# A convolution and expert kernel: the inverse step's imaginary sums, a second V buffer, later routing steps and an earlier gather

## The chip, the core and the metric

The kernel runs on one core of a Trainium2 chip. The metric is the device time of one execution in microseconds (us). Engines are named as in the profile: PE (TensorE, matmuls), DVE (VectorE), ACT (ScalarE), POOL (GpSimd), SP (the engine that issues most of the transfers here).

## What is computed

Eight batches of 3072 rows and 256 columns go through a circular convolution along the rows, done in the frequency domain. All 24576 resulting rows then go through a mixture of eight experts with a capacity each: a row goes to the expert of its largest logit, the first 768 rows of an expert (3072 / 8 * 2) are kept, and every other row of the output is zero.

```python
X = np.fft.rfft(x, axis=1)
Y = X * (filt_r + 1j * filt_i)[None, :, :]
x = np.fft.irfft(Y, n=3072, axis=1).reshape(B * S, D)
logits = x @ w_gate                      # 8 experts
expert_idx = np.argmax(logits, axis=1)
...
for i in range(N):                       # rows in order, capacity 768
    e = expert_idx[i]
    if counts[e] < capacity:
        disp[e, counts[e]] = x[i]
        ...
h = np.maximum(np.einsum('ecd,edf->ecf', disp, w1), 0.0)
y = np.einsum('ecf,efd->ecd', h, w2)
out[i] = gate_w[i] * y[expert_idx[i], pos[i]]      # kept rows only
```

## The kernel before, in words

**Two rounds, of which one counts.** The kernel first treats two and a half batches (t = 0, 1, 2; t = HALF = 2 is half a batch) and then all experts. Only where the experts are not full by then, a second round over the rest follows behind a branch; with this data it does not run.

**A stage** is the work of one t. It has eight steps h = 0 to 7, one for each group of four frequency pairs:

- *forward* (`pe_forward`, L475): 16 small matmuls of `wf` with `z_in` into PSUM banks 4 and 5 (`wide`);
- *multiply* (`dve_multiply`, L791): two DVE products of 128x1024 of `wide` with the filter `fab`, into `prod[:, n % 2, 0]` and `prod[:, n % 2, 1]`. The next forward waits for both (`p_done`), since `wide` is there once;
- *sums* (`dve_sums`, L797 and L799): a subtraction makes the real part in `prod[..., 0, :, 0, :]`, an addition the imaginary part in `prod[..., 0, :, 1, :]`;
- *inverse* (`pe_inverse`, L491) of the step before: 32 matmuls of 64x64 by 64x96 in four quadrants of PE, which accumulate real and imaginary part into PSUM banks 3 and 6 (`back`). It waits for both sums (`m_done`);
- *back* (`act_back`, L698): two ACT copies from `back` into `v_in`.

A matmul of `f32` shows as two records in the trace, so that a forward has 32 and an inverse 64; the transposes show once.

**Between them lies the work on the batch before** (`tok`): *logits* at h = 0 (`pe_logits`, L538), twelve *turns* of V, transposes on PE (`pe_turn_v`, L548) and ACT copies into `x_in` (L713), with *raw* (L558) after the second and *route in* (L569) after the fourth; twelve *products* (`pe_product`, L582) with ACT copies into `y` (L727) and stores of `y` to DRAM (`y_store`); thirty *route steps* on DVE (`dve_route`, steps 0 to 29 along `STEPS_BY`), among them the rank of step 10, which needs two matmuls (`pe_rank`, L593), and the table of step 28, which needs 24 matmuls (`pe_table`, L608) after step 27. The route ends in `dve_tokens` (L954 to L958), the row numbers by which the experts gather.

**Queues.** Every engine runs its instructions in the order of the code. SP issues the stores of `t_out` and `y`, the loads of `z_in` (`z_load`, into one of four buffers), the zeros of the output and the weights (`raw_load`), each behind a wait of its own. `first_raw`, the weights of the first expert, lie over `t_in`, and so does `t_out`.

**After the last stage** (`pe_last`, `act_last`, `dve_last`) the half batch is turned and multiplied. Its six rows of products take PSUM banks 0 to 3 (`place_of_row`); after the fourth comes the turn of the first gathered block (`pe_block_turn`, L646), and after the sixth `free_work` for all banks and then the rank.

**The experts** work through 16 blocks of 384 rows: *up* (L1267, 48 matmuls, into banks 4 to 7), *down* (L1281, 72 matmuls, banks 2 and 3), and before each up the *turn* of its block (L646), whose rows POOL gathers from DRAM (`pool_gather`, L1155). POOL issues in a fixed order: gathers, sends of the output (L1183) and the gates (L1167), with waits between (`pool_after` waits for an up to have come so far).

## Time and profile before

| | us |
|---|---|
| median of three runs | 492.42 |
| lowest and highest | 490.75 and 493.45 |
| the execution that was profiled | 491.62 |
| its span, first to last instruction | 489.8 |
| mean granted clock of TensorE, as a share | 0.989 |

Of the span PE is busy for 455.6 us, DVE for 233.4, ACT for 215.3 and POOL for 186.2. The span falls into a stage 0 (to 73.4 us), stage 1 (to 128), stage 2 (to 174), the last half batch (to 193) and the experts (to 484). A row of the timeline gives start and duration in us, the engine, the line of the code, the tile that is written and the ones that are read, shapes, count, and in brackets how long the engine sat idle before it and for whom.

### The profile page before, as it was taken

What the parts mean: (1) busy time and instruction counts of PE and PEld (TensorE: products, weight loads), DVE (VectorE), ACT (ScalarE), POOL (GpSimd) and SP (SyncE); (2) the same over time, 40 slices, a digit from 0 to 9 for tenths busy, and PEclk for the clock granted to TensorE, in tenths of its full rate; (3) what the DMA queues carried; (4) which work ended last, traced back from release to release, by engine and by line L of the source; (5) the groups of instructions that cost most, each with busy time, mean ns of one, the idle gap of its engine ahead of it and who ended that gap; (6) DMA issues with size and microseconds to landing.
All of it is one profiled execution on the core that took longest, in us unless ns stands there. A gap on an engine that the chain in (4) does not pass through costs nothing.

```text
span 489.8 us, 12096 instructions
## 1 busy us (share of the span) xinstructions
PE 455.6 (93%) x5160; PEld 400.8 (82%) x5160; DVE 233.4 (48%) x382; ACT 215.3 (44%) x402; POOL 186.2 (38%) x159
## 2 busy tenths in 40 slices
PE   5989999997898988999979999999999999999994
PEld 5855557555665574999979999999999999999993
DVE  2085535889399965870652242353134344224300
ACT  2745555452364555622634353455335345423310
POOL 0000000000000060467476787566786457583222
PEclk9999999998999999999989999999999999999998
DMA  8994989759854365733041894411795310970001
GB/s 297 412 403 131 337 257 336 277 206 332 286 166 163 139 225 141 258 98 98 22 141 45 277 387 154 140 44 34 260 399 179 131 43 24 347 276 23 33 34 38
DMA packets 45743, 93.00 MB, mean 190 GB/s; under 512 B 5840, under 2 KB 20848, under 8 KB 45168
## 3 DMA queue, kind: packets, MB, share of 16 engines
q1 hardware_dynamic: 39408, 79.48, 46.3%
q0 software_dynamic: 6272, 12.65, 7.7%
q8 instruction: 43, 0.70, 0.6%
q14 instruction: 20, 0.16, 0.1%
HBM read 46.47 MB, written 45.64 MB: 188 GB/s over the span
## 4 chain that ended last, share of the span: by engine, by line
PE 83%; DVE 10%; issue 3%; DMA 2%; ACT 1%; POOLq 0%; POOL 0%; SPq 0%; DVEq 0%; ACTq 0%
PE psum L1281 29%; PE psum L1267 25%; DVE prod L791 5%; PE psum L491 4%; PE psum L508 4%; PE psum L475 4%; PE psum L548 3%; PE psum L505 3%; PE psum L646 2%; PE psum L582 2%; PE psum L538 2%; PE psum L524 1%; DVE prod L799 1%; PE psum L578 1%; DMA g_in<-y_rows,token 1%
## 5 line engine op out<-in xcount | busy, mean ns | idle before, releaser
L1095 DVE SCALAR_TENSOR_TENSOR hl<-psum,hh 128x384 fp32r<-128x384 f32 x128 | 69.5, 555 | 145.7 <-ACT hh L1046 145.7
L1281 PE MATMUL psum<-w2h,hh 128*128 128x256 f32 x384 | 110.5, 288 | 0.0
L1281 PE MATMUL psum<-w2l,hh 128*128 128x256 f32 x384 | 109.3, 285 | 0.0
L1281 PE MATMUL psum<-w2h,hl 128*128 128x256 f32 x384 | 109.3, 285 | 0.0
L1046 ACT ACTIVATE hh<-psum 128x384 fp32r<-128x384 f32 x128 | 62.1, 492 | 60.8 <-PE psum L1267 60.0
L1267 PE MATMUL psum<-xh,w1h 128*128 128x384 f32 x256 | 86.1, 336 | 1.6 <-DVE hl L1095 1.5
L1267 PE MATMUL psum<-xh,w1l 128*128 128x384 f32 x256 | 85.6, 334 | 0.0
L1267 PE MATMUL psum<-xl,w1h 128*128 128x384 f32 x256 | 85.6, 334 | 0.0
L791 DVE TENSOR_TENSOR prod<-psum,fab 128x1024 f32<-128x1024 f32 x48 | 56.5, 1217 | 49.7 <-PE psum L475 41.9
L1183 POOL DMA_INDIRECT out<-o_out,token x48 | 49.2, 1025 | 74.0 <-ACT o_out L1055 60.1
L1281 PEld LDWEIGHTS psum<-w2l,hh 128*128 128x128 f32 x384 | 74.4, 194 | 0.0
L1281 PEld LDWEIGHTS psum<-w2h,hl 128*128 128x128 f32 x384 | 74.3, 193 | 0.0
L1281 PEld LDWEIGHTS psum<-w2h,hh 128*128 128x128 f32 x384 | 74.3, 193 | 0.0
L1055 ACT ACTIVATE o_out<-psum,o_gate 128x256 f32<-128x256 f32 x48 | 22.8, 476 | 108.3 <-PE psum L1281 108.3
L1155 POOL DMA_INDIRECT g_in<-y_rows,token x48 | 53.5, 1114 | 41.7 <-DVE token L958 26.8
L1167 POOL DMA_INDIRECT o_gate<-gate_rows,token x48 | 48.7, 1014 | 35.1 <-PE psum L1267 21.5
L1146 POOL DMA_DIRECT2D gate_rows<-gate x2 | 1.3, 660 | 145.6 <-DVE carry L893 145.6
L1267 PEld LDWEIGHTS psum<-xh,w1h 128*128 128x128 f32 x256 | 48.1, 188 | 2.5 <-DVE hl L1095 2.1
L1267 PEld LDWEIGHTS psum<-xl,w1h 128*128 128x128 f32 x256 | 48.1, 188 | 0.0
L1267 PEld LDWEIGHTS psum<-xh,w1l 128*128 128x128 f32 x256 | 48.1, 188 | 0.0
L491 PEld LDWEIGHTS psum<-wbi,prod 64*64 64x64 f32 x1536 | 33.9, 135 | 14.6 <-issue 8.8
L491 PE MATMUL psum<-wbi,prod 64*64 64x96 f32 x1536 | 38.9, 249 | 4.8 <-issue 2.3
(111 smaller groups left out, 533.0 us busy)
## 6 DMA issues: line engine op xcount, KB each, us to landing
out<-zero SPq DMA_DIRECT2D x24, 1024.0 KB, 6.2
w_raw<-in_w SPq DMA_DIRECT2D x14, 1024.0 KB, 5.8
x_in<-in_x SPq DMA_DIRECT2D x18, 512.0 KB, 6.7
t_scratch<-t_out SPq DMA_DIRECT2D x24, 256.0 KB, 4.4
z_in<-t_scratch SPq DMA_DIRECT2D x32, 192.0 KB, 3.9
y_rows<-y SPq DMA_DIRECT2D x12, 512.0 KB, 2.8
fab<-in_fab SPq DMA_DIRECT2D x4, 1024.0 KB, 14.4
first_raw<-in_w SPq DMA_DIRECT2D x2, 1024.0 KB, 7.6
```

What stands on the lines that cost most here:

```text
L475: mm = nc.tensor.matmul(wide[q * QR:(q + 1) * QR, a, c, :], wf[part(a), NQ * h + q, c, :], z_in[part(a), n % ZB, q, :], start=True, stop=True)
L491: mm = nc.tensor.matmul(back[q][part(low), at:at + 2 * HR], prod[part(q), n % 2, 0, a, c, d:d + A1], wbi[part(q), j, a, c, :], start=(c == ...
L508: mm = nc.tensor.matmul(work[k][:, :], wa[:, :], x_in[:, c, 2 * h:2 * h + 2, :], start=True, stop=True)
L791: nc.vector.tensor_tensor(prod[:, n % 2, f], wide, fab[:, h, :, f, :].unsqueeze(2).to_broadcast([P, 2, 2, D]), ALU.mult).then_inc(p_done, 1)
L1046: nc.scalar.activation(hh[:, b % 2, f, :], ps[(2, 3, 6, 7)[f % 4]][:, 0:TOK], ACT.Relu).then_inc(hh_done, 1)
L1055: nc.scalar.activation(o_out[:, b % 2, s, :], ps[4 + (b * ST + s) % 2][:, 0:D], ACT.Copy, scale=o_gate[:, b % 4, s:s + 1]).then_inc(o_evac, 1)
L1095: nc.vector.scalar_tensor_tensor(out=hl[:, b % 2, f, :], in0=ps[(2, 3, 6, 7)[f % 4]][:, 0:TOK], scalar=0.0, in1=hh[:, b % 2, f, :].bitcast ...
L1155: nc.gpsimd.indirect_dma_start(out=g_in[:, b % 2, s, :], out_offset=None, in_=yd[0:have], in_offset=bass.IndirectOffsetOnAxis(ap=tokens_of ...
L1167: nc.gpsimd.indirect_dma_start(out=o_gate[:, b % 4, s:s + 1], out_offset=None, in_=gd[0:have], in_offset=bass.IndirectOffsetOnAxis(ap=toke ...
L1183: nc.gpsimd.indirect_dma_start(out=out, out_offset=bass.IndirectOffsetOnAxis(ap=tokens_of(r, b, s), axis=0), in_=o_out[:, b % 2, s, :], in ...
L1267: mm = nc.tensor.matmul(ps[(2, 3, 6, 7)[f % 4]][:, 0:TOK], wt[k][:, h, f * P:(f + 1) * P], xx[:, b % 2, h, :], start=(m == 0), stop=(m == 5))
L1281: mm = nc.tensor.matmul(ps[4 + (b * ST + s) % 2][:, 0:D], hx[:, b % 2, f, s * P:(s + 1) * P], wt[k][:, f, :], start=(f == 0 and m == 0), s ...
```

## The change

Six things are changed at once.

1. *Imaginary sums.* In stages 1 and 2 the groups h = 4, 5 and 6 do not make the imaginary sum on DVE. `prod[..., 0, :, 1, :]` and `prod[..., 1, :, 0, :]` stay apart, and the inverse of these groups has three terms in place of two: 48 matmuls, the third of which adds the second imaginary part with the same `wbi`.
2. *A second V buffer.* Batch t = 1 is written to `v_other`, over `t_in`. Its first copy waits until `t_out` of t = 2 has been stored, and the weights that lie in the same place (`first_raw`, `w1h0`) wait for all turns of that batch.
3. *Turns and products.* The turns move from h = 0 and 1 to h = 1, 2 and 3 (`TURNED`), the products to h = 2 to 6 in both stages (`PRODUCTS`). A product waits for its own turn and no longer for all twelve.
4. *Route steps.* They move later (`STEPS_BY`), the exponential to h = 2, the rank to h = 3 and the table from h = 7 to h = 6. At h = 7 nothing of the route is left.
5. *The last half batch.* Rows 4 and 5 of the products go to banks 4 and 5; the rank goes ahead of them, right behind the first block turn; the wait for the banks is now with the first two parts of the first up, and with the first down.
6. *Queues.* SP loads `z_in` 4 to 6 of the last stage first, then stores two rows of `y`, then loads the first weights, then `z_in` 7; ACT splits the first weights at h = 5 and not at h = 3. POOL gathers block 4 right behind the sends of block 1, ahead of the gates of block 2; before, that gather waited for the second part of the up of block 3.

PE in stage 1, steps 5 to 7, where the chain of waits runs over DVE before the change. L475 is the forward, L491 the inverse, L608 the table, L582 a product. Before:

```order
L475 MATMUL psum<-z_in,wf 32x256 x16
L491 MATMUL psum<-wbi,prod 64x96 x32
L475 MATMUL psum<-z_in,wf 32x256 x16
L491 MATMUL psum<-wbi,prod 64x96 x32
L475 MATMUL psum<-z_in,wf 32x256 x16
L491 MATMUL psum<-wbi,prod 64x96 x32
L608 MATMUL psum<-hot_hi,hot_lo 128x96 x24
L491 MATMUL psum<-wbi,prod 64x96 x32
```

The same steps after (L491, L508, L625 and L599 are forward, inverse, table and product there):

```order
L491 MATMUL psum<-z_in,wf 32x256 x16
L508 MATMUL psum<-wbi,prod 64x96 x48
L599 MATMUL psum<-x_in,wai 128x512 x3
L491 MATMUL psum<-z_in,wf 32x256 x16
L508 MATMUL psum<-wbi,prod 64x96 x48
L625 MATMUL psum<-hot_hi,hot_lo 128x96 x24
L599 MATMUL psum<-x_in,wai 128x512 x3
L491 MATMUL psum<-z_in,wf 32x256 x16
L508 MATMUL psum<-wbi,prod 64x96 x80
```

Six products and the longer inverses stand in these steps now, and the table comes one step earlier; the last row is the inverse of group 6 (48) and that of group 7 (32).

POOL at the start of the experts. L1155 is a gather of three parts, L1183 a send, L1167 the gates. Before:

```order
L1155 DMA g_in<-y_rows,token_79 128x256 x3
L1183 DMA out<-o_out,token_78 24576x256 x3
L1167 DMA o_gate<-gate_rows,token_79 128x1 x3
L1155 DMA g_in<-y_rows,token_79 128x256 x3
L1167 DMA o_gate<-gate_rows,token_79 128x1 x3
```

After (L1179, L1207 and L1191):

```order
L1179 DMA g_in<-y_rows,token_79 128x256 x3
L1207 DMA out<-o_out,token_78 24576x256 x3
L1179 DMA g_in<-y_rows,token_79 128x256 x3
L1191 DMA o_gate<-gate_rows,token_79 128x1 x6
```

The gather of block 4 has moved ahead of the gates of block 2, whose wait stood before it.

PE at the seam from the last half batch to the experts. L578 is a product of the half batch, L646 the turn of the first block, L593 and L594 the rank, L1267 the first up. Before:

```order
L578 MATMUL psum<-x_in,wai 64x512 x8
L646 MATMUL psum<-sq,g_in 128x128 x6
L578 MATMUL psum<-x_in,wai 64x512 x4
L593 MATMUL psum<-lg,tri_half 128x8
L594 MATMUL psum<-lg,sq 128x8
```

After (L595, L663, L610 and L611):

```order
L595 MATMUL psum<-x_in,wai 64x512 x8
L663 MATMUL psum<-sq,g_in 128x128 x6
L610 MATMUL psum<-lg,tri_half 128x8
L611 MATMUL psum<-lg,sq 128x8
L595 MATMUL psum<-x_in,wai 64x512 x4
```

The rank stands ahead of the last two rows of products.


The diff, cut to what changes the order, the work or a wait:

```diff
-EXP_STEP = 1
-RANK_STEP = 2
+EXP_STEP = 2
+RANK_STEP = 3
...
-STEPS_BY = [4, 8, 17, 23, 25, 27, 28, 30]
+STEPS_BY = [0, 5, 10, 22, 25, 28, 30, 30]
...
+TURNED = [0, 0, 4, 8, 12, 12, 12, 12, 12]
+PRODUCTS = [0, 0, 0, 2, 4, 6, 9, 12, 12]
...
+def summed(t, h):
+
+    return t == 0 or h not in (4, 5, 6)
...
+        v_other = sb("v_other", [P, DH, N2, P], over="t_in")
...
         def sp_last_stage(sp, t, r):
-            z_load(sp, t, ZB)
+            for g in range(ZB, NG - 1):
+                z_load(sp, t, g)
+            y_store(sp, t - 1, 0)
+            y_store(sp, t - 1, 1)
             raw_load(sp, r, 0, 0)
             raw_load(sp, r, 0, 1)
-            z_load(sp, t, ZB + 1)
-            z_load(sp, t, ZB + 2)
-            y_store(sp, t - 1, 0)
-            z_load(sp, t, ZB + 3)
-            for c in range(1, products(t - 1) // 2):
+            z_load(sp, t, NG - 1)
+            for c in range(2, products(t - 1) // 2):
                 y_store(sp, t - 1, c)
...
         def pe_inverse(pe, t, j):
...
+            terms = [(0, 0, 0), (0, 1, 1)] if summed(t, j) else [(0, 0, 0), (0, 1, 1), (1, 0, 1)]
             for h in range(DH):
                 for a in range(2):
-                    for c in range(2):
+                    for i, (f, c, to) in enumerate(terms):
...
-                                mm = nc.tensor.matmul(back[q][part(low), at:at + 2 * HR], prod[part(q), n % 2, 0, a, c, d:d + A1],
-                                                      wbi[part(q), j, a, c, :], start=(c == 0), stop=(c == 1))
+                                mm = nc.tensor.matmul(back[q][part(low), at:at + 2 * HR], prod[part(q), n % 2, f, a, c, d:d + A1],
+                                                      wbi[part(q), j, a, to, :], start=(i == 0), stop=(i == len(terms) - 1))
...
         def pe_product(pe, t, i, k):
-            pe.wait_ge(vt_evac, t * 12 + 12 if t != HALF else t * 12 + 2 * i + 2)
+            pe.wait_ge(vt_evac, t * 12 + i + 1 if t != HALF else t * 12 + 2 * i + 2)
...
-                    if h == NG - 1:
+                    if h == NG - 2:
                         pe_table(pe, tok, 7)
-                    for i in products_at(tok, h, t == last - 1):
+                    for i in products_at(r, tok, h, t == last - 1):
                         pe_product(pe, tok, i, next_work("pe"))
...
         def place_of_row(t, i, engine):
-            return 2 + (i - 4) if t == HALF and i >= 4 else next_work(engine)
+            return i if t == HALF and i >= 4 else next_work(engine)
...
                     pe_block_turn(pe, r, 0)
+                    pe_rank(pe, t, 5)
                 pe_product(pe, t, i, place_of_row(t, i, "pe"))
-            for k in range(WORK + 1):
-                free_work(pe, k)
-            if r == 0:
-                pe_rank(pe, t, 5)
+            if r > 0:
+                for k in range(WORK):
+                    free_work(pe, k)
...
         def act_back(act, t, g):
+            if t == 1 and g == 0:
+                for c in range(NCH):
+                    act.wait_ge(t_written[c], 2 * 32)
...
-                nc.scalar.copy(v_in[:, :, :, u:u + 8], back[q].rearrange("p (h x n) -> p h n x", h=DH, n=N2)).then_inc(v_evac, 1)
+                nc.scalar.copy(v_of(t)[:, :, :, u:u + 8], back[q].rearrange("p (h x n) -> p h n x", h=DH, n=N2)).then_inc(v_evac, 1)
...
-                if t == last - 1 and h == 3:
+                if t == last - 1 and h == NG - 3:
                     act_split(act, r, 0, 0)
...
-                                    ALU.subtract).then_inc(m_done, 1)
-            nc.vector.tensor_tensor(prod[:, n % 2, 0, :, 1, :], prod[:, n % 2, 0, :, 1, :], prod[:, n % 2, 1, :, 0, :],
-                                    ALU.add).then_inc(m_done, 1)
+                                    ALU.subtract).then_inc(m_done, 1 if summed(t, h) else 2)
+            if summed(t, h):
+                nc.vector.tensor_tensor(prod[:, n % 2, 0, :, 1, :], prod[:, n % 2, 0, :, 1, :], prod[:, n % 2, 1, :, 0, :],
+                                        ALU.add).then_inc(m_done, 1)
...
                 turned(sp, (FIRST if r == 0 else NB) - 1)
+                if r == 0:
+                    sp.wait_ge(vt_done, 12 * (FIRST - 1))
+                    sp.nop(nofuse=True)
...
             pool_sent(pool, r, 1)
+            pool_gather(pool, r, 4)
             pool_after(pool, r, 2, 6)
             pool_gates(pool, r, 2)
-            pool_after(pool, r, 3, 2)
-            pool_gather(pool, r, 4)
             pool_after(pool, r, 3, 7)
...
                     if n * FT + f >= 4:
                         pe.wait_ge(hl_done, n * FT + f - 3)
+                    elif n == 0 and f < 2:
+                        free_work(pe, 4 + f)
...
             up(1)
+            if r == 0:
+                for k in range(2, 6):
+                    free_work(pe, k)
             down(0, 0)
```

## Rows read from the trace of the kernel before

**Rows 1.** Two stages: PE, PEld, DVE, ACT, POOL busy, granted clock, DMA share, GB/s.

```profile
73.40:128.00 54.60, 46.84 (x1014) 31.91 (x1010) 40.60 (x65) 22.55 (x46) 0.74 (x1) 0.97 0.85 296
128.00:174.00 46.00, 42.64 (x947) 29.62 (x946) 41.69 (x70) 24.61 (x45) 0.57 (x1) 1.00 0.46 157
```

**Rows 2.** The chain that ended last, stage 1: start, duration, what.

```profile
74.49 2.77 PE psum L538 x93
...
77.96 0.41 PE psum L538 x3
...
90.77 1.06 issue
...
117.25 2.03 PE psum L475 x32
...
124.59 1.01 PE psum L475 x29
125.61 1.88 issue
...
128.10 2.76 PE psum L538 x96
```

**Rows 3.** The same chain: what one piece of PE work takes.

```profile
83.79 2.90 PE psum L548 x24
...
97.31 1.48 PE psum L491 x64
98.79 3.63 PE psum L582 x8
...
131.88 1.26 PE psum L558 x12
...
134.05 0.33 PE psum L569 x2
...
217.82 1.07 PE psum L608 x24
```

**Rows 4.** Timeline of DVE, stage 2 and the last half batch.

```profile
146.28 0.17 DVE L891 TENSOR_TENSOR base<-psum,carry 128x8 f32<-128x8 f32 x1
...
148.53 2.35 DVE L791 TENSOR_TENSOR prod<-psum,fab 128x1024 f32<-128x1024 f32 x2
...
151.52 0.69 DVE L799 TENSOR_TENSOR prod<-prod 128x512 f32<-128x512 f32 x1
...
153.63 0.69 DVE L924 TENSOR_TENSOR hot_lo<-digits,pairs 128x1024 bf16<-128x1024 bf16 x1
...
191.47 1.01 DVE L834 TENSOR_TENSOR xl<-psum,xh 128x384 fp32r<-128x384 f32 x2
```

**Rows 5.** The chain at the start of the experts.

```profile
192.03 0.59 ACT y L727
...
192.97 0.36 PE psum L593 x2
193.55 6.35 PE psum L1267 x36
...
247.24 4.93 DMA g_in<-y_rows,token
...
253.09 10.12 PE psum L1281 x72
...
272.18 8.62 PE psum L1281 x72
```

**Rows 6.** Timeline of POOL: the last send of block 1.

```profile
232.78 0.99 POOL L1183 DMA_INDIRECT out<-o_out,token  x1 [0.30 <-issue]
```

**Rows 7.** Timeline of PE: the turn of block 4.

```profile
252.21 0.87 PE L646 MATMUL psum<-sq,g_in 128*128 128x128 f32 x6 [2.50 <-DMA g_in<-y_rows,token]
```

**Rows 8.** Busy time, granted clock (seventh number), DMA share and GB/s behind that turn.

```profile
253.00:256.00 3.00, 3.00 (x19) 3.00 (x19) 1.54 (x3) 2.45 (x3) 2.08 (x4) 0.61 0.16 44
```

**Rows 9.** The page's DMA queues: packets, MB, share of 16 engines.

```profile
q8 instruction: 43, 0.70, 0.6%
```

More of the change, by code:

```diff
@@ L85, in gates_before, with turned_at, products_at @@
     return 16 * sum(2 if k == HALF else 1 for k in range(t))
-def turned_at(h):
+def turned_at(r, h):
+    if r == 0:
+        return range(TURNED[h], TURNED[h + 1])
     return range(6 * h, 6 * h + 6) if h < 2 else range(0)
-def products_at(t, h, last):
+def products_at(r, t, h, last):
+    if r == 0:
+        return range(PRODUCTS[h], PRODUCTS[h + 1])
     if last:
@@ L282, in build @@
         ps = [psum[:, i].rearrange("p k d -> p (k d)") for i in (0, 1, 4, 5, 2, 3, 6, 7)]
-        work = [psum[:, i].rearrange("p k d -> p (k d)") for i in range(WORK + 1)]
+        work = [psum[:, i].rearrange("p k d -> p (k d)") for i in range(6)]
         back = [psum[:, i].rearrange("p k d -> p (k d)")[:, 0:DH * 4 * HR] for i in (3, 6)]
@@ L445, in sp_last @@
                     zeros(sp, n)
-        held = [None] * (WORK + 1)
+        held = [None] * 6
         place_of = {"pe": 0, "act": 0}
@@ L617, in pe_stage @@
                         pe_logits(pe, tok, 1)
-                    for i in turned_at(h):
+                    for i in turned_at(r, h):
                         pe_turn_v(pe, tok, i)
@@ L749, in act_stage @@
                 if tok is not None:
-                    for i in products_at(tok, h, t == last - 1):
+                    for i in products_at(r, tok, h, t == last - 1):
                         act_rows(act, tok, i, next_work("act"))
```

10 lines of the change are left out of this document (7 added, 3 removed).

## The prediction

> **What bounds the kernel now.** I read the stages by their busy time first. In stage 1 PE is busy for 46.8 of 54.6 us and DVE for 40.6, in stage 2 PE for 42.6 and DVE for 41.7 of 46.0 [rows 1]: two engines of nearly equal load that take turns at waiting. The chain of waits says where. Up to about 109 us it runs over PE, then over DVE (multiply, sums, route steps) to the end of stage 1, and over DVE again through nearly all of stage 2. Three more things lie on it. PE pauses three times in stage 1 with "issue" as the reason: 0.70 us ahead of the row at 77.96, 1.06 at 90.77 and 1.88 at 125.61 [rows 2]. One forward at 117.25 takes 2.03 us [rows 2] where 1.0 is usual. Last, at the start of the experts, PE waits 2.50 us for the gather of block 4 [rows 7]. Behind 253 us PE runs without a gap, which leaves up and down alone there; this part of 231 us the change does not touch.
>
> **Prices.** All from one profiled execution of 491.62 us. On PE: a forward about 1.03 (29 of its 32 records in 1.01) [rows 2]; inverse 1.48, four products 3.63 with their start, so 0.86 each, six turns 2.90, so 0.48 each, raw 1.26, route in 0.33, table 1.07 [rows 3]; rank 0.5, from 192.97 to the up at 193.55 [rows 5]; logits 2.76, or 3.88 with the pause in them (2.77 + 0.70 + 0.41) [rows 2]. On DVE: from a multiply to the second sum 3.0 and 0.6 more for that sum (148.53 to 151.52) [rows 4]; route steps 10 to 16 take 2.25 (146.28 to 148.53), steps 17 to 21 1.5 (152.13, where that second sum ends, to 153.63) [rows 4].
>
> **The sums.** A group without the addition saves DVE 0.6 us. Its inverse has 96 records in place of 64: 1.48 x 1.5 = 2.22, so PE pays 0.74. Over six groups that is 3.6 us off DVE and 4.4 us onto PE. It is worth something only where DVE is late. With the new tables six products and the table stand in steps 5 and 6 and make PE the late one there, so I expect no gain from this edit: with plain sums the list below comes out 0.2 us shorter per stage.
>
> **Stage 1, step by step**, from its first forward at 73.47 (74.49 less 1.02). I take for each step the longer of the two engines.
> Step 0: forward and logits with the pause, 4.9. Step 1: forward, four turns, raw, route in, inverse, 1.03 + 1.9 + 1.26 + 0.33 + 1.48 = 6.0. Step 2: forward, four turns, inverse, two products, 6.15. Step 3: the same and the rank, 6.6. Step 4: DVE, which has 3.6 of multiply and sums and 3.75 of route steps behind forward 3, lets forward 5 start 4.6 after forward 4 (PE alone would need 4.25). Step 5: forward, the long inverse 2.22, three products 2.6, 5.85. Step 6: the same and the table, 6.9. Step 7: forward, the multiply 2.4, two sums 1.2 and the last inverse 1.5, with the waits between 6.25. Together 47.25, so the last inverse ends at 120.7. Before it ended at 124.59, where the next forward starts [rows 2]. The 3.9 us are made of about 1.3 from the better spread, 1.5 from the pause at 90.77 (1.06 and 0.4 of restart, as the first pause shows), which came where two inverses and a forward ran close together and now has turns between, and 1.0 from the forward of 2.03.
> For that last the row shows a forward at twice its time after PE had mostly waited for DVE; it is the lower of the two clock levels (1.2 against 2.4 GHz), and in the new order PE has six products and two long inverses just there.
>
> **Stage 2** starts with the pause of 1.88 inside its first forward; from 124.59 to 128.10 pass 3.5 us for 1.02 of work, so it costs 2.5 [rows 2]. I keep it. From the logits on, the same steps without a pause in them are 45.1; before it was 45.6 (128.10 to 173.7). Gain 0.5.
>
> **The pauses** are the term I know least. Between the first and the second lie 254 matmul records, between the second and the third about 5 x 127. Each record has a weight load beside it, and the queue named instruction moved 43 packets of 16 KB [rows 9]; so the pauses sit at the borders of 16 KB of PE's instructions. They come in stage 1, with the DMA share at 0.85, and none in stage 2 with 0.46 [rows 1]. Counted on through the new order, a border falls into logits again at the same place, and two fall close together at the seam, near the last inverse and in the logits of stage 2, while zeros are written. Ends: nothing (2.5 gained) and two pauses of the largest kind there (2.5 lost). I take what the nearest row shows, 2.5 once.
> The Trainium skill says otherwise: "Runtime: NRT & Kernel Launch", section Instruction fetch mechanics, has blocks of 16 KiB fetched ahead, mostly hidden. The trace agrees on the size of the blocks and not on the hiding. By that page no pause would be left, and the sum would be 3.6 us lower.
>
> **The second V buffer.** The first copy into it waits for the last store of `t_out`, issued at about 79 us and landed four to five later, near 83.5; the copy is due at 84.4. Cost nothing, up to 1 us if it lands late, and then turns and rows queue behind it on ACT.
>
> **SP and ACT.** `z_load` 0 for stage 2 now stands behind the store of the twelfth product: about 114.5 in place of 109.9, 4 to 6.5 us to land, against a forward due at 120.7. Nothing to 1 us. The first weights leave at about 147 in place of 130.7 and need 6 to 10 us; ACT wants them near 157, after the rows of step 5. Nothing. `z_load` 7 behind them has four steps of slack.
>
> **The last half batch.** The first up starts at 193.55, behind an ACT copy until 192.62 and the rank [rows 5]. Now the rank (0.5) comes before two products (1.9) that start at 190.1, so PE is done at 192.5; bank 4, which the first part of the up needs, is free at about 192.3. What is late next is `xl`, 191.47 + 1.01 = 192.5 [rows 4]. The up starts at 192.65: gain 0.9, ends 0 and 1.0.
>
> **The gather.** The last send of block 1 ends at 233.8 [rows 6]. Three parts at 1.3 each end at 237.7, and 4.93 us later, as before [rows 5], the rows are there at 242.7, long before PE asks at 249.7. The wait of 2.50 goes [rows 7]. The turn and the down behind it took 0.87 and 10.12 where 0.66 and 8.62 are usual [rows 5, 7], at a granted clock of 0.61 just there [rows 8], between the two levels; that came after the wait and goes with it, 1.7. Gain 4.2, ends 2.5 and 4.2. The gates of block 2 are behind the gather on POOL; they waited until 238.2 anyway.
>
> **Sum.** 3.9 + 0.5 + 0.9 + 4.2 = 9.5; 491.62 - 9.5 = 482.1. The profiled execution is 0.8 below the median of the runs (492.42); between the two bases I say 482.5.
>
> **The rivals.** (a) The pauses go: 1.1 + 2.5 less, 478.9. For it: none in stage 2 before. Against: DMA in stage 1 stays as full. 0.09. (This is the case of the Trainium skill's page above.) (b) The seam costs more, by a second pause, a late `z_load` 0 or the lower clock again: 2.5 to 4 us more, 485 to 486.5. For it: borders that are close together, zeros in the queues. 0.14. (c) The gather wait stays or comes back as another (gates, `xl` of block 4, weights): 4.2 more, 486.7. Against: 7 us of slack. 0.06. (d) The change as a whole gives nothing beyond 0.5%, both (b) and (c): about 490 to 492. 0.03. (e) Slower: the first weights. ACT splits them ahead of the rows and copies of steps 5 and 6. If they land behind 157, every us is one of stage 2, since forwards and inverses wait for these copies; from 167 on the whole gain is gone, and at 172, three times the usual landing, it gives 496. Against: 6 to 10 us to land in busier stretches. 0.02. The forecast, 480.5 to 484.5, has 0.66.
>
> **How the numbers follow.** The range goes from 479.5 (part of a) to 487 (b and most of c). About 0.5% (2.5 us) is what a measurement here can tell from no change. Faster by more than that: all but (d) and (e), 0.95; same 0.03; slower 0.02.
>
> **What the profile after would show.** Stage 1's last inverse at 120.7, the logits of stage 2 at 124.2, its last inverse at 169.4, the first up at 188.3, no wait at the turn of block 4. On PE no wait for DVE in steps 5 and 6; the long inverses at 2.2. Wrong I am if the forward at step 7 again runs at twice its time, if "issue" in stages 1 and 2 adds up to over 5 us, or if PE waits for `z_in`, `first_raw` or a gather.

## The result, and the profile after

The changed kernel took 486.30 us (median of four runs, 484.90 to 489.04) where the kernel before took 491.59 beside it (489.92 to 493.45). The ratio is 0.9894, with a 95% interval from 0.9853 to 0.9936: faster by 5.3 us, inside the range and in the direction forecast, but 3.8 us above the 482.5 that I gave. The profiled execution took 487.66, with a span of 485.8 where it was 489.8. Some executions of a kernel run slower at a lower granted clock (one copy of this one took 653.9 us); the ratios and intervals leave them out.

Four more copies of the changed kernel ran later, with ratios of 0.9939, 0.9928, 0.9912 and 0.9932. The gain is more likely 4 us than 5.

**Where the time went**, in the two profiled executions:

| stretch | before | after | moved by | forecast |
|---|---|---|---|---|
| first forward of stage 1 to the end of its last inverse | 51.1 | 47.15 | -4.0 | -3.9 |
| from there to the logits of stage 2 | 3.5 | 1.0 | -2.5 | 0 |
| stage 2, logits to the logits of the last half batch | 46.7 | 54.4 | +7.7 | -0.5 |
| last half batch, logits to the first up | 18.7 | 17.85 | -0.8 | -0.9 |
| wait and slow work at the turn of block 4 | 4.2 | 0 | -4.2 | -4.2 |

The rest (-0.4 ahead of stage 1) is within what two executions differ by. Three of the rows came as forecast. The seam and stage 2 together cost 5.2 us more, where I had 0.5 less. The first up starts at 193.43, as before at 193.55 [rows 5]: all that stage 1 and the last half batch had won is gone again by then, and only the gather's 4.2 us reach the end.

The stages of the changed kernel, to be held against [rows 1] (PE, PEld, DVE, ACT, POOL busy, granted clock, DMA share, GB/s):

```profile
73.00:121.00 48.00, 46.26 (x1114) 32.40 (x1106) 38.90 (x62) 22.41 (x46) 0.74 (x1) 1.00 0.73 245
121.00:138.00 17.00, 13.14 (x295) 10.41 (x283) 11.97 (x17) 6.74 (x15) 0.00 (x0) 1.00 1.02 327
138.00:175.00 37.00, 32.56 (x760) 21.39 (x759) 29.09 (x51) 18.18 (x31) 0.65 (x2) 1.00 0.47 159
```

In stage 1 PE is busy for 46.3 of 48.0 us: it is now the one engine that sets this stage, with DVE at 38.9, and the DMA share is lower than before. Then come 17 us in which PE is busy for 13.1 only and the DMA share is at 1.02.

The chain that ended last, over the seam and through stage 2 (start, duration, what), against [rows 2]:

```profile
118.67 1.55 PE psum L508 x64
120.22 1.02 PE psum L491 x32
121.25 1.02 PE psum L555 x29
122.27 2.43 issue
124.70 2.16 PE psum L555 x67
...
131.07 0.71 issue
...
137.28 1.65 issue
...
161.96 1.37 issue
...
193.43 6.50 PE psum L1292 x36
```

Four pauses of "issue" stand in stage 2, 6.16 us in all, where before none stood there; the whole program before had 3.64 us of them ahead of the experts [rows 2]. The forward that took 2.03 us [rows 2] takes 1.02.

What PE does between the first two of them (start, duration, engine, line, tiles, records, in brackets the idle time ahead and for whom):

```profile
124.70 2.16 PE L555 MATMUL psum<-v_other,wgs 128*32 128x128 f32 x67 [2.43 <-issue]
126.78 1.09 PE L491 MATMUL psum<-z_in,wf 64*32 64x256 f32 x32
127.81 1.09 PE L565 MATMUL psum<-sq,v_other 128*128 128x128 f32 x8
128.74 1.42 PE L575 MATMUL psum<-nums,lg_t 128*128 128x32 f32 x12
130.00 1.07 PE L565 MATMUL psum<-sq,v_other 128*128 128x128 f32 x8
131.78 0.59 PE L586 MATMUL psum<-lg_u,wai 128*128 128x192 f32 x2 [0.71 <-issue]
```

67 + 32 + 8 + 12 + 8 = 127 records; from the second pause to the third it is 126, from the third to the fourth 504, which is four times 126. These are the borders of 16 KB found in the prediction from the distances before and from the queue that moved 43 packets [rows 9]; now it moved one more:

```profile
q8 instruction: 44, 0.72, 0.6%
```

The traces show more than these rows. Counted over all recorded instructions of PE (weight loads, matmuls and waits), the four pauses stand 256, 256 and 1024 instructions apart, to within one. In the 14 profiles of this study there are 50 such rows of "issue" ahead of the experts, and 49 of them lie on one grid of 256 instructions (the 50th is in e1 below). The traces also have the time of every packet of the queue named instruction, and one packet belongs to each border. In the changed kernel (us; a border is named by its place in PE's recorded instructions):

| border | PE enters the block before it | packet starts | packet has landed | PE is at the border | PE goes on | DMA share until the packet starts |
|---|---|---|---|---|---|---|
| 4289, in the logits | 116.7 | 122.28 | 123.23 | 122.27 | 124.70 | 1.00 |
| 4545 | 124.7 | 129.21 | 130.16 | 131.07 | 131.78 | 1.05 |
| 4801 | 131.8 | 136.16 | 137.38 | 137.28 | 138.92 | 1.02 |
| 5057 | 138.9 | 140.01 | 141.12 | 145.55 | at once | 0.02 |
| 5825, in a long inverse | 155.9 | 160.65 | 161.74 | 161.96 | 163.33 | 1.01 |
| 6081 | 163.3 | 164.45 | 165.41 | 169.70 | at once | 0.14 |

At each of the 49 pauses PE goes on 1.2 to 1.8 us after its packet has landed, and at every border of stages 1 and 2 that PE passed without one, the packet had landed at least 1.07 us before. So a pause is the time by which a packet comes too late. What makes it late is its start: with a DMA share under 0.2 in the first us behind PE's entry it started at most 1.6 us after it, and with the queues full up to 6.2 us after it.

What fills the DMA queues just there is SP's doing. Its issues around the seam (start, duration; `zero` is a store of 1 MB of zeros):

```profile
115.11 0.99 SPq L389 DMA_DIRECT2D z_in<-t_scratch  x2
116.14 0.54 SPq L396 DMA_DIRECT2D out<-zero  x1
...
118.61 1.32 SPq L396 DMA_DIRECT2D out<-zero  x1
...
122.15 1.55 SPq L396 DMA_DIRECT2D out<-zero  x1
...
125.50 1.12 SPq L396 DMA_DIRECT2D out<-zero  x1
126.72 1.50 SPq L389 DMA_DIRECT2D z_in<-t_scratch  x2
```

Before, the same four stores left from 111.9 to 122.3. They stand behind the stores of `y`, those stand behind the products, and the products have moved later while stage 1 has become shorter. So the 4 MB of zeros now fall between the seam and step 1 of stage 2.

The gather: its three parts on POOL end at 237.7, and PE's turn of block 4 no longer waits, against [rows 6] and [rows 7].

```profile
236.74 1.00 POOL L1179 DMA_INDIRECT g_in<-y_rows,token  x1 [0.30 <-issue]
```

```profile
249.58 0.82 PE L663 MATMUL psum<-sq,g_in 128*128 128x128 f32 x6
```

The down behind it starts at 250.40 and takes 8.63 us where it took 10.12 [rows 5].

### The profile page after: what moved, and what is told of

Same layout as the page of the kernel before. It is cut to its first block, busy times and chain, and to the rows that moved or that the text cites. A ratio compares the mean times of both kernels' runs of the same rounds, so it can differ in the third digit from the quotient of the medians.

```text
span 485.8 us, 12483 instructions
## 1 busy us (share of the span) xinstructions
PE 456.1 (94%) x5352; PEld 401.8 (83%) x5352; DVE 230.2 (47%) x376; ACT 215.3 (44%) x402; POOL 185.9 (38%) x159
## 3 DMA queue, kind: packets, MB, share of 16 engines
q1 hardware_dynamic: 39408, 79.48, 46.9%
## 4 chain that ended last, share of the span: by engine, by line
PE 69%; DVE 3%; issue 2%; ACT 1%; POOLq 0%; ACTq 0%
PE psum L1306 28%; PE psum L1292 26%; PE psum L508 3%; PE psum L565 2%; PE psum L599 2%; PE psum L663 2%; PE psum L491 2%; PE psum L555 1%; DVE w1l L1041 1%; DVE hot_lo L945 1%; PE psum L575 1%; DVE prod L811 0%; PE psum L625 0%; ACT w1h L1031 0%; PE psum L595 0%
## 5 line engine op out<-in xcount | busy, mean ns | idle before, releaser
L1207 POOL DMA_INDIRECT out<-o_out,token x48 | 48.9, 1019 | 68.2 <-ACT o_out L1079 53.2
L1179 POOL DMA_INDIRECT g_in<-y_rows,token x48 | 53.4, 1113 | 46.8 <-issue 45.9
L1191 POOL DMA_INDIRECT o_gate<-gate_rows,token x48 | 48.6, 1012 | 37.4 <-PE psum L1292 23.4
L1292 PEld LDWEIGHTS psum<-xh,w1h 128*128 128x128 f32 x256 | 48.1, 188 | 3.6 <-DVE hl L1119 2.1
L508 PEld LDWEIGHTS psum<-wbi,prod 64*64 64x64 f32 x1728 | 37.3, 133 | 15.6 <-issue 10.8
L508 PE MATMUL psum<-wbi,prod 64*64 64x96 f32 x1728 | 42.6, 246 | 7.1 <-issue 3.7
L1292 PEld LDWEIGHTS psum<-xl,w1h 128*128 128x128 f32 x256 | 48.1, 188 | 0.0
L1292 PEld LDWEIGHTS psum<-xh,w1l 128*128 128x128 f32 x256 | 48.1, 188 | 0.0
```

The costliest lines, as they stand in the source:

```text
L508: mm = nc.tensor.matmul(back[q][part(low), at:at + 2 * HR], prod[part(q), n % 2, f, a, c, d:d + A1], wbi[part(q), j, a, to, :], start=(i = ...
L1179: nc.gpsimd.indirect_dma_start(out=g_in[:, b % 2, s, :], out_offset=None, in_=yd[0:have], in_offset=bass.IndirectOffsetOnAxis(ap=tokens_of ...
L1191: nc.gpsimd.indirect_dma_start(out=o_gate[:, b % 4, s:s + 1], out_offset=None, in_=gd[0:have], in_offset=bass.IndirectOffsetOnAxis(ap=toke ...
L1207: nc.gpsimd.indirect_dma_start(out=out, out_offset=bass.IndirectOffsetOnAxis(ap=tokens_of(r, b, s), axis=0), in_=o_out[:, b % 2, s, :], in ...
L1292: mm = nc.tensor.matmul(ps[(2, 3, 6, 7)[f % 4]][:, 0:TOK], wt[k][:, h, f * P:(f + 1) * P], xx[:, b % 2, h, :], start=(m == 0), stop=(m == 5))
```

## The theories

**Theory A.** The lost time is the pauses: PE's own instructions arrive late at the borders of 16 KB when the DMA queues are full and PE goes through small matmuls quickly. Then moving the zeros moves the pauses, and another number of PE instructions moves the borders.

**Theory B.** It is the longer inverses: the six groups cost PE time where PE is the late engine, and the pauses would be there anyway. Then plain sums give several us back.

**Theory C.** Stages 1 and 2 don't matter at all, since something else sets the first up (the weights, the route), and the whole result is the gather.

"Stage 1" below is from its first forward to the logits of stage 2, "stage 2" from there to the logits of the last half batch, "pauses" the sum of "issue" on PE from the first forward of stage 1 to the first up; these three come from the one profiled execution of each kernel, in us. The ratio is to the kernel before on the same chip, with its 95% interval.

| kernel | ratio | stage 1 | stage 2 | pauses |
|---|---|---|---|---|
| before | 1 | 54.6 | 46.7 | 3.64 |
| after, first result | 0.9894 [0.9853, 0.9936] | 48.1 | 54.4 | 6.16 |
| r0_after | 0.9939 [0.9905, 0.9974] | 49.1 | 52.1 | 4.72 |
| e1_plain_sums | 0.9935 [0.9886, 0.9983] | 50.1 | 50.7 | 5.23, of which 3.27 at borders |
| e2_no_seam_zeros | 0.9859 [0.9798, 0.9919] | 49.0 | 50.2 | 2.86 |
| e3_zeros_early | 0.9918 [0.9880, 0.9955] | 52.7 | 49.1 | 1.83 |
| r1_after | 0.9928 [0.9899, 0.9957] | 49.8 | 53.0 | 6.27 |
| e4_gather_alone | 0.9923 [0.9897, 0.9950] | 51.4 | 47.4 | 1.23 |
| e5_zeros_late | 0.9980 [0.9947, 1.0012] | 54.1 | 48.5 | 4.05 |
| e6_zeros_in_experts | 0.9887 [0.9839, 0.9936] | 48.4 | 50.6 | 3.14 |
| r2_after | 0.9912 [0.9878, 0.9946] | 50.6 | 52.5 | 6.71 |
| e8_interleaved | 0.9887 [0.9833, 0.9941] | 48.7 | 51.4 | 4.25 |
| e9_shifted | 0.9932 [0.9905, 0.9960] | 49.2 | 53.3 | 5.99 |
| e10_interleaved_plain | 0.9863 [0.9815, 0.9911] | 49.7 | 49.7 | 2.20 |

The first four experiments ran on a chip on which every kernel is some 18 us slower (before: 509.99); only their ratios and their places are compared with the rest.

## Experiments on the first chip: the sums and the zeros

**r0_after** is the changed kernel, unchanged, as the ground to stand on.

> The changed kernel again, as the base for the other three on this chip. Both theories: 484.5 to 488, ratio to the kernel before 0.985 to 0.993. Theory P (pauses): the trace again has pauses of PE with reason issue in stage 2, their sum between the first forward of stage 1 and the first up 4 to 8 us, and stage 1 itself 47 us long. Theory C (chance): the pauses of the profiled run were an accident; this time they add up to under 3 us and stage 2 is near 46 us.

Measured: 507.26 us, ratio 0.9939. Its pauses stand at the same records as in the first result, with other lengths: 2.07 in the logits, 0.17, 0.28, 1.40 in the long inverse, and 0.80 in stage 1 that the first result did not have. Their sum of 4.72 is in the range expected; stage 1 is 2 us longer than expected.

**e1_plain_sums** undoes the first edit alone.

```diff
-    return t == 0 or h not in (4, 5, 6)
+    return True
```

> The changed kernel with both sums on DVE in all groups and inverses of 32 matmuls, nothing else changed. Theory P: PE is the late engine in steps 5 and 6, so the time falls by 0.4 us (0.2 per stage by the step sum), or by 1 to 3 us where 96 fewer small matmuls also move or spare a refill of PE's instructions. Rival D (the sums on DVE are what matters): slower by 1 to 3.6 us, the six additions of 0.6 us.

Measured: ratio 0.9935, not told apart from r0. The two intervals leave room for 2 us either way, so that the time alone doesn't decide on theory B; the stages do, below. What the plain sums change is where the pauses are:

```profile
127.75 0.62 PE L491 MATMUL psum<-z_in,wf 64*32 64x256 f32 x4 [0.96 <-issue]
...
160.74 0.38 PE L508 MATMUL psum<-wbi,prod 64*64 64x96 f32 x2 [0.79 <-issue]
...
180.01 1.49 PE L575 MATMUL psum<-nums,lg_t 128*128 128x32 f32 x6 [1.96 <-issue]
```

The pause of the logits has gone into the forward behind them. Before, it came after 29 of 96 records; now it comes 67 + 28 = 95 records later. Ahead of it three inverses of stage 1 have 32 records less each, 96 in all. So the places of the pauses hang on the count of instructions and not on what an instruction does or waits for.

The third row is of another kind. It lies on no border (302 records behind the second), and PE goes on at 180.01, when ACT's second copy into `lg_t` ends (179.48 and 0.48), ahead of which ACT had stood still for 3.46 us. So this was a wait for ACT, though the row says "issue", and 3.27 us are left at borders. What ACT waited for is not shown.

Against the list in the prediction: without its pauses stage 1 is 0.3 us longer than r0's and stage 2 0.7 us, since PE's wait for the sums ahead of the last inverse grows from 1.7 to 2.4 us. I had plain sums 0.2 us shorter per stage. Theory B, by which plain sums would give several us back, falls with this: without the pauses both stages are longer, not shorter, and so they are in e10 against e8 below (0.6 and 0.7 us).

**e2_no_seam_zeros** leaves the four stores of zeros at the seam out.

```diff
             for g in range(ZB):
                 z_load(sp, t + 1, g)
-                if r == 0:
-                    zeros(sp, NG - 1 - ZB + g)
...
-            pool.wait_ge(first_zeroed, 16 * FIRST_ZEROS)
+            pool.wait_ge(first_zeroed, 16 * (FIRST_ZEROS - ZB))
```

> The changed kernel without the four zero stores of 1 MB that SP issues among the loads for stage 2; four of the 24 blocks of zeros are never written. Theory P: the pauses of PE at the seam and in the first half of stage 2 (2.43, 0.71 and 1.65 in the profiled run, with restart about 6 us) go, the pause at 162 behind the first weights stays: 479.5 to 482. Rival C: within 1 us of the changed kernel. Rival Z (z_in is what is late): pauses stay, and waits for z_in were hidden in them.

Measured: 502.49 us in the median, ratio 0.9859, some 4 us below r0, though the intervals overlap. The DMA share over 121 to 138 us, and PE's rows of "issue":

```profile
121.00:138.00 17.00, 15.71 (x369) 12.46 (x370) 13.20 (x20) 8.32 (x18) 0.00 (x0) 1.00 0.54 118
```

```profile
124.32 2.16 PE L553 MATMUL psum<-v_other,wgs 128*32 128x128 f32 x67 [1.29 <-issue]
...
159.46 1.04 PE L506 MATMUL psum<-wbi,prod 64*64 64x96 f32 x34 [0.87 <-issue]
```

The second and third pause of stage 2 are gone with the full queues. The one in the logits is there, with 1.29 us, and so is the one at the long inverse. That does not speak against A: over 117 to 124 us the loads of `z_in` keep the share at 1.03 in this kernel too, and over 154 to 157 the first weights (issued at 147) keep it at 0.98. The packets say the same: those of these two borders start 4.04 and 4.40 us after PE enters the block before, those of the two whose pause is gone 2.18 and 1.00.

**e3_zeros_early** puts them between the stores of `y` of stage 1.

```diff
                 y_store(sp, t - 1, c)
+                if r == 0 and 1 <= c <= ZB:
+                    zeros(sp, NG - 2 - ZB + c)
...
-                if r == 0:
-                    zeros(sp, NG - 1 - ZB + g)
```

> The changed kernel with the same four zero stores issued between the stores of y in steps 3 to 5 of stage 1, so that all the work is done. Theory P: they drain before the dense stretch at the seam, which loses its pauses; a store or two of y and z_in 7 land later, hidden. 480.5 to 483.5. Rival: the zeros take the transfers' time wherever they are, new pauses in steps 4 to 7 of stage 1 take the place of the old: 485 to 488.

Measured: ratio 0.9918, 1 us below r0 and not told apart from it, where 3 to 6 us less than the changed kernel were expected. Only 1.83 us of pauses are left, none of them between 79 and 162 us, which is what A says. But a new wait took their place (waits of PE, in us in total, times, longest):

```profile
PE psum L491 <- DMA z_in<-t_scratch: 2.9, 1, 2.9
```

All four loads of `z_in` for stage 2 now stand behind 4 MB of zeros and the `y` rows, and the forward of stage 2 waits for one. This wait is also why the border in the logits brings no pause here: its packet lands at 125.33, as late as in the other copies, but PE is there only at 127.75.

## Experiments on the second chip: which part brings the gain

**r1_after** again is the changed kernel.

> The changed kernel again, as the base for this call. Ratio to the kernel before 0.985 to 0.995. Theory P: issue pauses ahead of the first up add up to 4 to 7 us, most of them behind the first forward of stage 2.

Measured: 488.04 us, ratio 0.9928.

**e4_gather_alone** is the kernel before with the gather of block 4 moved, and nothing else.

```diff
             pool_sent(pool, r, 1)
+            pool_gather(pool, r, 4)
             pool_after(pool, r, 2, 6)
             pool_gates(pool, r, 2)
-            pool_after(pool, r, 3, 2)
-            pool_gather(pool, r, 4)
```

> The kernel before with the gather of block 4 moved ahead of the gates of block 2 and nothing else. Theory: all of it is kept, minus 4.2 us (the wait of 2.5 and the slower clock behind it, 1.7), ratio 0.991 to 0.992; the trace has no wait at the turn of block 4 and 8.6 us for the down behind it. Rival (the clock would have fallen anyway, by the wait of 1.0 for hl just before): minus 2.5, ratio 0.995. So if the whole change gives 0.989 to 0.994, stages 0 to 2 and the last half batch together give next to nothing, as the trace after says.

Measured: 488.03 us, ratio 0.9923. This one move gives what the whole change gives. The turn of block 4 has no wait ahead of it:

```profile
246.55 0.82 PE L646 MATMUL psum<-sq,g_in 128*128 128x128 f32 x6
```

That is 0.77% or 3.8 us, beside the 4.2 forecast. All the other edits together gave nothing in time on this chip that could be told from zero. C is right as far as the sum goes, but not in its reason: stage 1 did become shorter, by 4.0 us in the mean (five copies of the changed kernel: 49.4; the three profiles with the old order, before, e4 and e5: 53.4), and stage 2 longer by 6 (53.1 against 47.0 in before and e4). The first up moves when either moves: 190.6 in e6 below, 193.9 in r1. The profiled execution of e4 was the fastest of its eleven (485.12, median 488.03), so its 1.23 us of pauses are the low end of what this order has; before and e5 have 3.64 and 4.05.

**e5_zeros_late** does to the kernel before what the change did to it by the way: it moves the same zeros into stage 2.

```diff
             for g in range(ZB):
                 z_load(sp, t + 1, g)
-                if r == 0:
-                    zeros(sp, NG - 1 - ZB + g)
...
         def sp_last_stage(sp, t, r):
+            if r == 0:
+                for g in range(ZB):
+                    zeros(sp, NG - 1 - ZB + g)
             z_load(sp, t, ZB)
```

> The kernel before with one thing changed: the four zero stores of 1 MB that SP issues among the first loads for stage 2 are issued behind them, ahead of z_in 4 and the first weights, so that the same bytes fall into stage 2. Theory P (full queues starve PE's instructions in dense code): the pause at the seam (1.88) shrinks or goes, and pauses come up between 128 and 145 us, 2 to 4 in all: time between 1 us less and 3 us more than the kernel before, with pauses in stage 2 where it had none. Rival N (the pauses come from the new order of PE's instructions alone): no pause in stage 2.

Measured: 490.75 us, ratio 0.9980 with 1 inside the interval. The pause at the seam, 1.88 us in [rows 2], is gone, and one stands in stage 2, which had none:

```profile
141.59 0.38 PE L492 MATMUL psum<-wbi,prod 64*64 64x96 f32 x3 [1.74 <-issue]
```

```profile
128.00:142.00 14.00, 12.26 (x243) 10.68 (x242) 10.19 (x18) 7.79 (x16) 0.00 (x0) 1.00 1.03 342
```

PE's program is the same as before, instruction for instruction. From the border at the seam to this one it is 3 + 96 + 8 + 12 + 8 + 2 + 8 + 32 + 24 + 61 = 254 records, twice 127. So the border was there all along; in the profile of before PE ran through it. Its packet starts 1.55 us after PE enters the block before it in the profile of before, and 6.2 us after in e5. It is the one pause that came up in stage 2. (The one near 90 us is 1.88 here, where before had 1.06.) For the time, one pause took another's place. (In e4, whose zeros are where they were, that border took 0.57.)

**e6_zeros_in_experts** is the changed kernel with these zeros issued among the expert weights.

```diff
             for g in range(ZB):
                 z_load(sp, t + 1, g)
-                if r == 0:
-                    zeros(sp, NG - 1 - ZB + g)
...
+                if q == 0 and r == 0:
+                    for g in range(ZB):
+                        zeros(sp, NG - 1 - ZB + g)
                 if q > 0 and r == 0:
```

> The changed kernel with the same four zero stores behind the third expert's first weights, where PE runs 128x384 matmuls and needs few instructions; all the work is done. Theory P: as without those zeros at all, 3 to 6 us less than the changed kernel, ratio to the kernel before 0.979 to 0.985, stage 2 below 48 us. Rival: the output sends wait for the zeros on POOL, gates and gathers behind them come late, and the gain is given back there: ratio 0.99.

Measured: 486.27 us, ratio 0.9887, beside 0.9928 for r1 with overlapping intervals; 0.979 to 0.985 and a stage 2 below 48 us were expected, and the rival had 0.99. Stage 2 is 2.4 us shorter, the pauses at 131 and 137 us are gone, and those in the logits (2.14) and the long inverse (0.85) stay. The first up starts at 190.61, 3.3 us ahead of r1, but the time is only 1.8 us less: the sends on POOL wait 6.2 us for the zeros, and PE gets a new wait of 1.5 us for `g_in` at 224.8, as the rival said.

## Experiments on the third chip: a better place for the zeros

**r2_after** is the changed kernel once more.

> The changed kernel, as the base for this call. Ratio to the kernel before 0.986 to 0.994. If only the order of the code counts, the pauses come at the same records as in the two traces so far (in the logits of stage 2 after 29 of 96 records, in the inverse after 12 of 64, in a long inverse after 62 of 96).

Measured: ratio 0.9912. Its four pauses, 6.71 in all, are at records seen in the earlier copies: in stage 1, in the logits, in the inverse and in the long inverse. The one at 131 us is missing this time; there the packet had landed 1.22 us before PE came.

**e8_interleaved** issues the loads of `z_in` and the zeros for stage 2 in pairs behind the stores of `y` in steps 4 to 7, so that they are spread over the end of stage 1.

```diff
-            turned(sp, t + 1)
-            for g in range(ZB):
+                if r == 0 and c >= 2:
+                    if c == 2:
+                        turned(sp, t + 1)
+                    z_load(sp, t + 1, c - 2)
+                    zeros(sp, NG - 1 - ZB + c - 2)
+            if r > 0:
+                turned(sp, t + 1)
+            for g in range(ZB if r > 0 else 0):
                 z_load(sp, t + 1, g)
-                if r == 0:
-                    zeros(sp, NG - 1 - ZB + g)
```

> The changed kernel with the four z_in loads for stage 2 and the four zero stores spread over steps 4 to 7 of stage 1, each pair behind a store of y, in place of all of them behind the last store; nothing else moves, all the work is done. Theory P: the queues are drained by about 125 in place of 137, so the pauses in steps 1 and 2 of stage 2 go and the one in its logits shrinks: 2 to 5 us less than the changed kernel, ratio to the kernel before 0.982 to 0.988. Rival Q (it is the bytes, not when they come): pauses of the same sum, now in steps 5 to 7 of stage 1, 0 to 1 us.

Measured: 485.40 us, ratio 0.9887, just outside the 0.982 to 0.988 expected and with an interval that overlaps that of r2. The share over 73 to 121 us rises to 0.90, over 121 to 138 it falls to 0.59. As in e6, two pauses are gone and two stay:

```profile
126.02 2.15 PE L559 MATMUL psum<-v_other,wgs 128*32 128x128 f32 x67 [2.70 <-issue]
```

```profile
130.00:140.00 10.00, 10.00 (x204) 8.02 (x202) 9.15 (x16) 6.55 (x15) 0.00 (x0) 1.00 0.32 82
```

From 130 to 140 us PE does not stand still once, with the DMA share at 0.32; in r2 the same ten us have 9.2 us of work and a share of 0.99. At the border in the logits the share is 1.01 (117 to 124 us) in e8 too; its pause did not shrink, against what was expected, but is the longest of the study, with a packet that starts 5.53 us after PE enters the block before.

**e9_shifted** was to move every border by 64 records with 64 empty instructions at the start of PE's program.

```diff
+            for _ in range(64):
+                pe.nop(nofuse=True)
             pe.wait_ge(wa_loaded, 16)
```

> The changed kernel with 64 empty instructions on PE ahead of everything, where PE waits for x_in anyway. If the pauses sit at the borders of 256-instruction blocks, each comes 64 instructions, some 32 matmul records, earlier in the code: the one in the logits of stage 2 (after 29 records) moves to the end of the forward before them, the one in the long inverse from record 62 to about 30. If they belong to a place or to a moment of the transfers alone, they stay at their records. Time within 2 us of the changed kernel either way.

Measured: ratio 0.9932, pauses at the very same records. But the trace has 12483 instructions, as many as that of the changed kernel, and of the same kinds. The traces show no empty instruction anywhere, so that the count alone does not prove that the 64 are gone; with the grid of 256 that every other profile keeps, unmoved pauses say so too. I take this as a fifth copy of the changed kernel, in which a shift by empty instructions was not tried. What stands for A's second half is the grid in all profiles and its place in e1 and e10.

**e10_interleaved_plain** is e8 with the plain sums of e1.

```diff
-    return t == 0 or h not in (4, 5, 6)
+    return True
```

> The interleaved kernel with both sums on DVE in all groups, as the candidate for the fastest. Step sum: 0.4 us less than the interleaved one. Rival: the additions are late on DVE once the pauses are gone, 0.5 to 1.5 us more.

Measured: 485.12 us, ratio 0.9863. It has the lowest ratio of the kernels that do all the work: by the ratios 6.7 us below before (0.0137 x 492) and 2.4 below r2, though its interval and that of r2 overlap. Against e8, which differs by the sums alone, it is 1.2 us shorter by the ratios and 0.3 by the medians, and neither can be told from zero. The border has moved as in e1, from 29 records into the logits to 28 records into the forward behind them:

```profile
127.64 0.62 PE L495 MATMUL psum<-z_in,wf 64*32 64x256 f32 x4 [1.34 <-issue]
```

It costs 1.34 us there and 2.70 in e8. Plain sums have a price of another kind in this trace and in that of e1. PE waits longer for DVE at the end of stage 2, and then runs slowly (first two rows of PE, then the windows, in which the granted clock is the third number from the end):

```profile
168.74 2.43 PE L512 MATMUL psum<-wbi,prod 64*64 64x96 f32 x64 [2.36 <-DVE prod L824]
172.13 4.71 PE L559 MATMUL psum<-v_in,wgs 128*32 128x128 f32 x96 [0.96 <-ACT v_in L722]
```

```profile
168.50:172.00 3.50, 2.43 (x64) 2.14 (x64) 3.46 (x7) 0.78 (x2) 1.86 (x1) 0.60 0.00 0
172.00:177.00 5.00, 4.87 (x98) 4.38 (x99) 1.61 (x1) 0.64 (x3) 4.09 (x4) 0.59 0.92 321
```

In e8 the wait is 1.71, the inverse takes 1.55 and the logits 2.8 at a clock of 1.00. At about 0.6 the mean clock is between its two levels of 1.2 and 2.4 GHz; inverse and logits took 2.8 us more by it. In e1 the same inverse has the same wait of 2.37 ahead of it, and the clock is 0.63 over 169 to 173.6 us. That the wait brings the lower clock is not shown: both kernels have a wait of 2.37 ahead of the last inverse of stage 1 too, and there the clock stays at 1.00.

## Why the prediction was right, and where it was not

**Direction and range** held, and so did four of its steps.

*The gather.* 4.2 forecast, 4.2 in the trace, 3.8 as the ratio of e4. The wait, the slow turn and the slow down went together, as said.

*Stage 1.* The step list gave 47.25 to the last inverse, the trace 47.15. The two are closer than the list deserves. It counted a pause of 1.1 us in the logits that this execution didn't have, and the four other copies had (0.80 to 2.35); less these pauses and a restart of 0.4 they come to about 46.9, where the list without its pause has 46.15. The steps are 0.7 to 1.0 us too short (47.15 is without a pause), and the mean gain of 4.0 us over five copies fits by that luck. The slow forward went: the clock over 117 to 124 us is 0.76 in before, e4 and e5, with the old order, and 1.00 in every profile that has the new one.

*The last half batch.* 0.9 forecast, 0.8 measured, limited by `xl`, as said.

*The sums.* "I expect no gain from this edit" held as far as it can be measured: e1 and r0, and e10 and e8, are not told apart. Its working was off by up to 1 us per stage, on the side of the longer inverses.

**The step that failed** is the pauses in stage 2: "They come in stage 1, with the DMA share at 0.85, and none in stage 2 with 0.46", "I take what the nearest row shows, 2.5 once". The mechanism behind it was the right one, the borders of 16 KB and the full queues, and I even counted "two fall close together at the seam, near the last inverse and in the logits of stage 2, while zeros are written". The term was mis-sized: -0.5 for seam and stage 2 together, +5.2 in the trace. Stage 2 took 54.4 us where 46.2 were forecast. Of these 8.2 us 6.2 are four pauses and 1.1 their restarts, 0.3 to 0.4 each at three of them; 0.9 are left over, in no single wait. (The restarts show in e6 and e8: with two pauses less, stage 2 less its pauses takes 47.6 us, and 48.2 in the changed kernel.) The seam itself gave 2.5 back, since the pause moved out of it.

The cause of the mis-sizing is that I read the DMA share of 0.46 as a property of stage 2. It was a property of the order on SP. I costed SP's new order by whether a load arrives in time ("Nothing to 1 us", "Nothing") and not by what else runs while 4 MB of zeros and 2 MB of weights pass. Both had moved: the zeros from 111.9-122.3 to 116.1-125.5, on PE work that starts 4 us earlier, and the first weights from 130.7 to 150.3, ahead of the border at 162. Loads and stores of data were in time everywhere, as forecast. What was late were the packets of PE's own instructions: at the four borders they started 4.4 to 5.6 us after PE had entered the block before, and PE was through with that block in 5.5 to 6.4 us.

The condition under which I would be wrong was named: over 5 us of "issue" in stages 1 and 2. It was 6.16. Of the rivals it was (b), seam costs more, and in the profile beyond its price: 5.7 us more than forecast where I had 2.5 to 4. I gave it 0.14. The profiled execution is 1.4 us above the median of its runs, and so 486.30 still lies inside the 485 to 486.5 of (b). As for the Trainium skill, "Runtime: NRT & Kernel Launch", section Instruction fetch mechanics: blocks of 16 KiB agree with 126 to 127 records between the places, in every copy. That their fetch is mostly hidden does not agree with the changed kernel, 4.7 to 6.7 us in five copies; it agrees better with the fastest run of e4, where 1.2 us are left.

**What stays open.** That full queues make the pauses is shown by experiment at the borders at 131 and 137 us: there they come and go with the zeros in e2, e6, e8 and, the other way round, in e5. At the border in the logits and at the one near 160 us the queues were full in every variant of the new order, by loads of `z_in` and by the first weights; there it rests on the times of the packets, which start as late as at the other two, and no kernel with these queues empty was run. The length of one pause changes between executions of one kernel (0.28 to 1.65 at the same record, in r0 and the first result), and a full queue does not always bring one. Over 154 to 160 us e10 has a share of 1.06 and 0.98 and no pause: its packet had landed at 157.71, and PE reached the border at 159.48. Why a packet starts 1.5 us after PE's entry one time and 5 us another, both with full queues, is not known from these runs. Nor is it known what PE does in the 1.2 to 1.8 us after the landing. How much of the 4 us between two kernels' single profiles is chance can't be said; the table's ratios are what carries weight, and by them none of the three new places for the zeros is told apart from the changed kernel. The first weights issued as early as before, with all else changed, were not run.

## What to carry to other kernels

Borders at which an engine may run out of instructions lie at fixed counts of its instructions, also where the profile of before shows no pause; so count them through the new order, and look at each for what the DMA queues carry at that time afterwards, not before. Bulk transfers that nobody waits for (zeros here) are not free: each row of "issue" that they brought here was gone when they moved, though what that gives in time is at the edge of what these runs can tell. And when one of several edits has an effect of its own that is easy to price, run it alone first: here one move on POOL was the whole gain.

## What the runs showed of the hardware

- The places where PE can pause with "issue" as the reason lie 256 recorded instructions apart (126 to 127 small matmuls, each with its weight load); 49 pauses of 0.15 to 2.70 us in 14 profiles. A change of 96 records moved such a place by 95.
- One packet of 16 KB in the queue named instruction belongs to each block. PE went on 1.2 to 1.8 us after it had landed. It started at most 1.6 us after PE's entry into the block before with a DMA share under 0.2 in the first us, and up to 6.2 us after it with a share near 1.0.
- Such a pause costs up to 0.4 us more behind it, in the restart: three records of a logits take 0.41 us.
- The same kernel, the same record: from 0.28 to 1.65 us between executions. Five copies of one kernel had ratios from 0.9894 to 0.9939.
- Of two chips with the same kernels, one was slower by 3.6% (509.99 against 492.27 for the kernel before), and the ratios stayed the same within their intervals (0.9939 and 0.9928).
- PE's clock was at 0.60 over an inverse and the logits behind it after waits of 2.36 and 0.96 us (e10), and at 1.00 after waits of 1.71 and 0.98 (e8) and after a wait of 2.37 at the end of stage 1 (e10 and e1).
- A row of "issue" is not always the engine's own: in e1 one of 1.96 us ended when a copy on ACT did.
